# GpSimd splits the experts' weights in 256-element pieces for every unit, not only for the first two

## The reference

```
x = attention(q, k, v), window 128, batch 4, heads 8, seq 576, head_dim 64   # -> (2304, 512)
h = x @ w_in; r = maximum(h, 0); x = (r * r) @ w_out                         # 512 -> 2048 -> 512
logits = x @ w_gate                                                          # (2304, 8)
P = exp(logits - logits.max())
for _ in range(8):
    P /= P.sum(1, keepdims=True) + 1e-9
    P /= P.sum(0, keepdims=True) + 1e-9
    P *= N / E
out = 0
for e in range(8):
    h = maximum(x @ w1[e], 0)                                                # 512 -> 1024
    out += P[:, e:e+1] * (h @ w2[e])                                         # 1024 -> 512
```

## Time and profile before

| what | value |
|---|---|
| median of three runs | 2151.76 us |
| the profiled execution's own time | 2151.85 us |
| its span, first to last instruction | 2150.1 us |
| TensorE (PE) busy | 2104.8 us, 98% |
| TensorE weight loads (PEld) busy | 1901.9 us, 88% |
| VectorE (DVE) busy | 1365.4 us, 64% |
| ScalarE (ACT) busy | 589.6 us, 27% |
| GpSimd (POOL) busy | 987.5 us, 46%, in 716 instructions |
| mean granted TensorE clock | 0.994 of full speed |
| chain that ended last | PE 92%, DVE 5%, issue 1%, ACT 1% |

### The profile page before, as it was taken

How to read it: one execution, slowest core, us unless ns; L and a number is a source line. 1 busy time by engine, 2 the same in 40 slices (tenths; PEclk the granted TensorE clock), 3 DMA queues, 4 the chain that set the end, 5 groups by cost and what they waited for, 6 DMA issues and landing times.

```text
span 2150.1 us, 39546 instructions
## 1 busy us (share of the span) xinstructions
PE 2104.8 (98%) x13270; PEld 1901.9 (88%) x13270; DVE 1365.4 (64%) x3012; ACT 589.6 (27%) x1609; POOL 987.5 (46%) x716
## 2 busy tenths in 40 slices
PE   7899999999999899999999999999999999999999
PEld 3789898889998789989998998899899899989988
DVE  7576675675657766666666666766666666666665
ACT  5565565564521211111111111211111111111111
POOL 3222222224573355455545545564554555455451
PEclk9999999999999999999999999999999999999999
DMA  5232333322211111111111111121111111111111
GB/s 127 63 88 61 100 81 83 87 72 72 83 48 30 40 40 50 41 48 47 41 49 39 49 42 46 47 83 52 40 49 39 49 44 44 49 39 49 42 46 54
DMA packets 165123, 121.05 MB, mean 56 GB/s; under 512 B 64400, under 2 KB 129936, under 8 KB 165008
## 3 DMA queue, kind: packets, MB, share of 16 engines
q1 hardware_dynamic: 165008, 119.59, 19.5%
HBM read 114.84 MB, written 4.72 MB: 56 GB/s over the span
## 4 chain that ended last, share of the span: by engine, by line
PE 92%; DVE 5%; issue 1%; ACT 1%; DMA 0%; SPq 0%; DVEq 0%; ACTq 0%
PE bank L781 35%; PE bank L725 33%; PE bank L664 9%; PE bank L657 9%; PE bank L622 2%; PE bank L648 2%; PE bank L633 1%; ACT prob L875 1%; DVE relu L1129 1%; DVE row L1163 1%; DVE g1l L1098 0%; PE bank L593 0%; DVE xl L1112 0%; DVE acc L1240 0%; DVE prob L1056 0%
## 5 line engine op out<-in xcount | busy, mean ns | idle before, releaser
L1247 DVE SCALAR_TENSOR_TENSOR acc<-bank,gate,acc 128x512 f32<-128x512 f32 x531 | 398.7, 751 | 285.3 <-PE bank L781 283.5
L725 PE MATMUL bank<-xh,eh 128*128 128x288 f32 x1792 | 532.0, 297 | 0.5 <-DVE u L1213 0.5
L725 PE MATMUL bank<-xl,eh 128*128 128x288 f32 x1792 | 530.6, 296 | 0.0
L725 PE MATMUL bank<-xh,el 128*128 128x288 f32 x1792 | 528.5, 295 | 0.0
L781 PE MATMUL bank<-fh,gh 128*128 128x512 f32 x1152 | 451.0, 391 | 0.7 <-DVE acc L1240 0.4
L781 PE MATMUL bank<-fh,gl 128*128 128x512 f32 x1152 | 450.8, 391 | 0.0
L781 PE MATMUL bank<-fl,gh 128*128 128x512 f32 x1152 | 450.6, 391 | 0.0
L725 PEld LDWEIGHTS bank<-xh,eh 128*128 128x128 f32 x1792 | 337.9, 189 | 3.3 <-DVE u L1213 0.7
L725 PEld LDWEIGHTS bank<-xl,eh 128*128 128x128 f32 x1792 | 338.1, 189 | 2.6
L725 PEld LDWEIGHTS bank<-xh,el 128*128 128x128 f32 x1792 | 339.0, 189 | 0.0
L483 POOL TENSOR_TENSOR wl<-stage,wh 128x512 fp32r<-128x512 f32 x120 | 161.2, 1344 | 367.3 <-ACT wh L843 367.3
(11 more groups left out here) (132 smaller groups left out, 3000.4 us busy)
## 6 DMA issues: line engine op xcount, KB each, us to landing
fw<-in_moe_w_dram SPq DMA_DIRECT2D x64, 512.0 KB, 3.6
stage<-in_moe_w_in_dram SPq DMA_DIRECT2D x64, 256.0 KB, 3.1
stage<-in_moe_w_out_dram SPq DMA_DIRECT2D x64, 256.0 KB, 2.7
ew<-in_moe_w_dram SPq DMA_DIRECT2D x64, 256.0 KB, 2.8
a<-in_moe_w_dram SPq DMA_DIRECT2D x64, 128.0 KB, 2.6
ew<-in_moe_w_dram SPq DMA_DIRECT2D x64, 128.0 KB, 2.7
k_raw<-in_k_dram SPq DMA_DIRECT2D x32, 128.0 KB, 2.6
q_raw<-in_q_dram SPq DMA_DIRECT2D x32, 128.0 KB, 2.5
```

The costliest lines, as they stand in the source:

```text
L725: done = pe.matmul(ps[:, 0:BH], w[r][:, a, kc, :], x[:, j, b, kc, :], start=(first and kc == 0 and w is eh and x is xh), stop=(kc == 1 and ...
L1247: dve.scalar_tensor_tensor(out=z, in0=ps, scalar=weight, in1=z, op0=ALU.mult, op1=ALU.add).then_inc(z_free, 1)
```

## The change

The condition `V < 2` is taken away, and with it the four whole-tile instructions. Every unit now prepares its weights as units 0 and 1 did: seven copies and seven subtractions of 256 elements for the first layer, four and four for the second. The last instruction of each group carries the semaphore, as in units 0 and 1.

```
--- before.py
+++ after.py
-                if isinstance(V, int) and V < 2:
-                    for a in range(OPS):
-                        last = pool.tensor_copy(eh[r][:, a, :, :], raw[:, a, :, :])
-                    last.then_inc(e_chain, 1)
-                    ...
-                    last.then_inc(f_split, 1)
-                    return
-                pool.tensor_copy(eh[r][:, :, :, :], raw[:, :, :, :]).then_inc(e_chain, 1)
+                for a in range(OPS):
+                    last = pool.tensor_copy(eh[r][:, a, :, :], raw[:, a, :, :])
+                last.then_inc(e_chain, 1)
                 wait_alone(pool, e_chain, done + 5)
-                pool.tensor_tensor(el[r][:, :, :, :], raw[:, :, :, :], low, ALU.subtract).then_inc(e_split, 1)
+                for a in range(OPS):
+                    last = pool.tensor_tensor(el[r][:, a, :, :], raw[:, a, :, :], low[:, a, :, :], ALU.subtract)
+                last.then_inc(e_split, 1)
                 wait_alone(pool, f_in[r], pairs * 16 + 16)
-                pool.tensor_copy(fh[r][:, :, :], fw[r][:, :, :]).then_inc(e_chain, 1)
+                for c in range(2):
+                    for h in range(2):
+                        at = slice(h * 2 * P, (h + 1) * 2 * P)
+                        last = pool.tensor_copy(fh[r][:, c, at], fw[r][:, c, at])
+                last.then_inc(e_chain, 1)
                 wait_alone(pool, e_chain, done + 6)
-                pool.tensor_tensor(fl[r][:, :, :], fw[r][:, :, :], f(fh[r][:, :, :]), ALU.subtract).then_inc(f_split, 1)
+                for c in range(2):
+                    for h in range(2):
+                        at = slice(h * 2 * P, (h + 1) * 2 * P)
+                        last = pool.tensor_tensor(fl[r][:, c, at], fw[r][:, c, at], f(fh[r][:, c, at]), ALU.subtract)
+                last.then_inc(f_split, 1)
```

## The result

The changed kernel takes 2137.36 us (median of six runs, 2134.41 to 2139.16) against 2150.59 us for the kernel before on the same chip (six runs, 2147.81 to 2154.64). The ratio is 0.9936, 95% interval 0.9922 to 0.9949: by this ratio 13.8 us faster, between 11 and 17. The forecast was 2136 us, counted from 2151.8 us, so a gain of 16.

The account below looks back on a forecast made before the run. The prediction took TensorE as the bound, stopped three times by gate steps waiting for GpSimd. From 2151.8 us it took 17.9 - 0.4 - 1.4 = 16.1 us, giving 2136 us, range 2133.5 to 2142.5.

Parts of the forecast that it names:

- The place and the mechanism: Gate steps in units 1 to 3: VectorE waits for whole GpSimd instructions holding the shared port, stopping TensorE; 10.2 us waited.
- 17.9 us gross: Cost of all three TensorE stops with their slow clock: 5.5 us for the first, 12.4 for the others.
- 0.4 for tile 8: Tile 8 waits for tile 5's addition, 0.1 to 0.2 us three times, 0.4 us in all.
- 1.4 for the late additions: TensorE waits 0.7 us for VectorE's late additions after tile 8, in units 1 and 2; 1.4 us together.
- sizing by unit pace: Second and third stops sized from unit 2 to unit 4: 13.64 us surplus over plain units, less 1.2, gives 12.4.
- 1.1 us of waits on subtractions after tile 7: VectorE's three steps after tile 7 wait on GpSimd's subtraction pieces: 0.35, 0.33 and 0.40 us, bounds 0 and 2.1.
- rival of two pieces: VectorE gets its turn only after two GpSimd pieces, bringing stops and later additions; 2143 us, chance 0.07.
- that of no entry: VectorE isn't let in until GpSimd's row of pieces ends, each stop 1.6 us longer; 2156.7 us, chance 0.05.
- clock rival: A 0.7 us TensorE wait already brings the low clock, 1.7 us each, twice; 2139.4 us, chance 0.11.
- L1175 below 0.7 us: Sign expected in the changed kernel's profile: this VectorE gate step, 1.07 us before, stays below 0.7 us.
- TensorE's two waits on the additions: Sign expected in the new profile: TensorE's L725 waits twice for VectorE's L1213 or L1216, 0 to 1.7 us each.
- 155: Sign expected in the new profile: GpSimd busy 155 us more, 62 x 2.5, with no TensorE wait on it.

Follow-up runs that it names:

- e3: Kernel before, GpSimd's instructions whole, the gate's small row and column vectors in PSUM instead of SBUF; 2134.97 us, ratio 0.9922.
- e1: Kernel before with pieces for units V = 0 to 3 only, whole tiles later; 2148.24 us, ratio 0.9976.
- e2: Kernel before with only the first layer's subtraction in pieces, in every unit; copies and second layer whole; 2137.02 us, ratio 0.9934.
- e7: Kernel before with the first layer's copies and subtractions in two instructions each, second layer whole; 2144.7 us, ratio 0.9963.
- e9: Kernel e3 with 9 unused VectorE reductions added to the gate step after tile 4; 2146.65 us, one execution.
- e10: Kernel e3 with 12 unused VectorE reductions added to the gate step after tile 4; 2144.05 us, one execution.
- e5: The changed kernel run again, unaltered, against the kernel before; 2137.71 us, ratio 0.9925.
- e8: Kernel e3 with 6 unused VectorE reductions added to the gate step after tile 4; 2140.34 us, one execution.

## Why the prediction was right

**The place and the mechanism.** Right, and shown: e3 takes the wait away with GpSimd untouched, e1 one stop at a time, e2 and e7 by size. L1154's longest is 0.75 us against 3.69 for L1163 before. The cause is shown for the steps and for the stretch, not for the clock.

**The sum.** I had 17.9 us gross, 0.4 for tile 8, 1.4 for the late additions, 16.1 net. The stretch saved 16.3 in the first profile and 17.3 in the second (67.36). e3, where nothing waits, saved 17.5; that is the gross figure measured, 0.4 under mine. The sizing by unit pace held because the low clock followed all three stops in the profile of before; e9 and e10 show that it need not. That 16.1 and 16.3 lie so close is in part luck: the gross figure was 0.4 us too high, the 1.4 us of late additions didn't come, and 0.5 us came that I had not counted (below). And the whole execution gained 13.2 us by the medians and 13.4 in the profile, not 16: the medians of before were 2151.8 in the forecast and 2150.59 here, and the rest was lost ahead of the stretch.

**The step that was mis-sized** is the 1.1 us of waits on subtractions after tile 7, and the 1.4 us of TensorE waiting that followed from it. VectorE's steps there took 2.57 us against 2.31 without waits: 0.26, not 1.1. L1201 of unit 2 came 676.89 - 674.14 = 2.75 us into the hidden part, 0.95 late instead of 1.9. By my own sum the second addition then ends at 1.80 + 0.95 + 0.97 = 3.72 us, ahead of the sixth product at 3.99, and there is no wait on L716 at all. The term for tile 8 was too large as well: 0.54 us between tiles where 0.37 is usual, so 0.17 us. One subtraction in its row of the kernel after, the one in progress when L1154 asked at 674.82 (columns: duration ns min/median/max, first and last start):

```profile
L541 POOL TENSOR_TENSOR el<-ew,eh x1: 853/853/853, 674.2 to 674.2; 128x256 fp32r<-128x256 f32 x1
```

It began at 674.19, just behind L1166 (674.14), took 0.85 us instead of the 0.74 that is the median of 21 such pieces, and ended at 675.04; L1154 ended at 675.08. So here L1166 met no piece that held it up (0.31 us), and L1154 asked late in the next one. I had counted 0.35 for the first step and full remainders of 0.33 and 0.40 us for the other two, from the moment they start. They lost 0.00, 0.08 and 0.18 us. A step's own time is not added to the wait: L1154's end lies 0.04 us behind the piece's, though alone it takes 0.18.

**A cost that I missed.** In unit 1 the gate step after tile 1 met L530 and L532, which are 256-element instructions in both kernels: L1154 took 0.75 us and L1156 0.72, and TensorE's L781 after tile 4 came late. These four rows show it, kernel after, VectorE and then TensorE:

```profile
665.20 0.75 DVE L1154 TENSOR_SCALAR row<-row 128x18 f32<-128x18 f32 x1
...
666.28 0.72 DVE L1156 TENSOR_TENSOR gate<-gate,row 128x144 f32<-128x144 f32 x1
```

```profile
667.23 0.39 PE L772 MATMUL bank<-fh,gl 128*128 128x512 f32 x1
...
668.12 0.50 PE L772 MATMUL bank<-fh,gh 128*128 128x512 f32 x1 [0.21 <-DVE acc L1231]
```

0.89 us lie between these two matmuls, where 0.37 is usual: 0.5 us lost. Before, the same two steps took 0.21 and 0.49 us (L1163 at 662.33 in the earlier trace rows, L1165 behind it). The same two steps in the repeat, kernel e5:

```profile
667.28 0.17 DVE L1154 TENSOR_SCALAR row<-row 128x18 f32<-128x18 f32 x1
667.78 0.47 DVE L1156 TENSOR_TENSOR gate<-gate,row 128x144 f32<-128x144 f32 x1
```

There the two steps are short and the stretch is 1.0 us shorter, of which this accounts for 0.5: it depends on where GpSimd happens to be. A step of 18 elements can lose a whole small instruction by asking just too late: L529 ended at 665.22, but L530 had begun at 665.17, and L1154, asking at 665.20, waited until L530 was over.

**The rivals.** VectorE is let in between adjoining pieces: in the eight row steps and eight column steps of the kernel after, and those of e5, no instruction on `gate` or `row` took longer than 0.83 us, of which 0.31 are the step's own, so none waited longer than one piece of 0.74. That ends both the rival of two pieces and that of no entry. The row on L1163 at 662.33 in the earlier trace rows pointed that way before the run, but it was one instance, and L1154 at 665.20 above shows that such a gap can be missed. The clock rival didn't come up in the changed kernel, as no wait of 0.7 us arose; in e8 three waits of that length were not followed by the low clock. Pieces in units 4 and on cost nothing: 1411.8 us from there to the end before, 1411.7 after. Of the signs the prediction named, L1175 below 0.7 us held in the first profile (0.59) and not in e5 (0.83), TensorE's two waits on the additions didn't come, and GpSimd's 151 us more stand against 155.

## What to carry to other kernels

When a tiny VectorE step takes microseconds, lay GpSimd's timeline beside it: if the two end within 0.2 us of each other every time (0.03 and 0.16 us here), it most likely waited for a whole GpSimd instruction, and the longest such instruction near a serial chain sets the price, whatever the averages say. Either cut that instruction to pieces shorter than the slack of the chain (here 0.7 us pieces against 1 us; two halves of 2.4 and 1.9 us saved 9.8 us of the stretch instead of 16.3), or let the small operands live in PSUM so that the step doesn't need the port, which costs GpSimd nothing (986.9 us busy in e3, 987.5 before) and was at least as fast. Then ask what the stop had been covering: here VectorE's work after tile 7 became the next thing in line: of 3.99 - 1.80 - 0.97 = 1.2 us of room in unit 1 it used 0.95. And split the trace at points that no edit touches before trusting a total: here everything ahead of the stretch moved by some us from one execution to the next, and everything behind it by 0.1.

## What the runs showed of the hardware

VectorE is let in between two GpSimd instructions that follow without a gap: seven times 256 elements, start to start 0.70 us where nothing interferes, and no instruction of a gate step longer than 0.83 us beside them (0.75 in the kernel after, 0.83 in e5), against 3.69 us beside one instruction of 4.01. GpSimd takes up the next instruction 0.04 to 0.05 us before the last has ended (665.17 and 665.22), and the one step that asked in between, at 665.20, waited for the next one too. A `reciprocal` from SBUF to SBUF took 0.27 us in every gate step of the kernel after, beside GpSimd's pieces too, and the reduction over rows 0.30. A subtraction in pieces took up to 0.85 us where a gate step had begun just before it, and 0.74 in the median; that it waited for VectorE in turn is likely and not shown. Small pieces cost GpSimd 2.48 to 2.72 us against 1.69 for the copies and 4.87 to 5.11 against 4.01 for the subtractions.

The granted clock was 0.50 behind some stops and stayed at 1.00 behind others. By the wait at the small matmul: up to 0.9 us (e2, e8) it was 1.00 each time; from 1.2 to 1.45 us (e7) it fell once of three, at 1.7 us (e9) twice of three, at 2.7 us (e10) once of three, and from 3.2 to 3.7 us (before, e1) five times of five. It also fell, in all twelve profiles, during or behind forty matmuls of eight columns, with TensorE busy throughout.
